# Attention stage of a fused kernel: another order of work on four engines, sinks masked after the turn, one copy moved to VectorE

## Chip, core and metric

One core of a Trainium2 chip. The metric is the time of one execution on the device in microseconds (us), the median of three runs.

## The reference

Three layers follow one another: attention with sinks and a sliding window, a dense layer with a cosine gate, and a top-1 mixture of experts. Only the attention is touched.

```python
# q, k, v: (4, 8, 768, 64); n_sink = 4, window = 128
scores = q @ k.T / sqrt(D)
keep = (key < n_sink) | ((query - key >= 0) & (query - key < window))
a = exp(where(keep, scores, -1e9) - rowmax); a = a / (a.sum() + 1e-9)
attn = a @ v
# then x: (3072, 512) -> dense (512 -> 2048 -> 512) -> 8 experts (512 -> 1024 -> 512)
```

## The kernel before

The 32 heads are taken as 16 pairs. A pair has 6 blocks of 128 queries (QB = 6), one step each; an iteration `it` is two pairs, 12 steps, and there are 8. Since the window is 128, a block of queries sees its own block of keys, the block before, and the sinks: 32 columns of the first keys. The two blocks complement each other: where a key of the own block lies ahead of the query, the same column of the block before is in the window. So both are joined into one block of 128 columns; block 0, which has none before it, takes a filler of -1e30 (`unseen`).

For step n, block n, both heads:

- PE `scores(n)` (L1518, L1519): four products (q by k_hi and k_lo for two heads) into `twin[n % 2]`. It waits for the exponentials of step n-2.
- DVE `join_scores(n)`: one predicated copy into the twin (L1073) and the row maximum (L1075).
- ACT `exponentials(n)`: neg_max (L783) and two exponentials into `probs` (L791).
- PE `turn_probs(n)`, two steps later (TURN_LAG): two transposes (L1527); behind an odd block also `turn_sinks` (L1532), one transpose for the sinks of two blocks, into the third part of `X_BANK`.
- DVE `copy_probs(n)` (L1083): the turned block times the two triangles `halves_of`, which takes the joined block apart again.
- ACT `copy_sinks(m)` for odd m (L798): the turned sinks to `sink_probsT`.
- PE `weigh_window(n)`, three steps later (PV_LAG, L1548): eight products with v (four in block 0), and for odd blocks `weigh_sinks` (L1555), which waits for `copy_sinks`.
- DVE `scale_o(m)` for odd m, four steps later (L1091 to L1096), then PE `turn_o(m)` (L1565) and ACT `stage_x(m)` (L806), five steps later.

Beside this, the next pair's q and k are split into a high and a low part, in four parts: 0 and 2 are halves of q, 1 and 3 halves of k. ACT makes the high part in `split_part` (L777, L779), POOL the low part (L621, L623). POOL also fills the sink columns of k (`fill_sinks`, L606 to L610) ahead of parts 0 and 2, for the k half 1 and 3; ACT's high part of k waits for that fill. The table `PARTS` says in which step of a pair ACT takes which part.

Each engine works through its list in program order. All waits are semaphores written by hand. The waits that matter here:

```python
# PE, turn_sinks(m): x_stage of the group before last
at_least(pe, x_staged, group(it, m) - 1)
# PE, weigh_sinks(m)
pe.wait_ge(sinksT_made, group(it, m) + 1)
# ACT, split_part, for a part of k
act.wait_ge(sinks_filled, 2 * (2 * it + i) + c // 2 + 1)
```

A group is two blocks, so the first one makes turn_sinks(m) wait for stage_x(m-4), which ACT makes in its step m+1, while PE turns the sinks of m in step m+2.

Of the kernel before, what the change touches and what calls it, by code (L numbers as in the profile page):

```python
# [20 lines left out]
U32 = mybir.dt.uint32  # L21
# [18 lines left out]
def build_program(nc, q_twice, k_twice, kT, v, config, w_dense, modality, w_gate, w_gate_rows, modality_bias, w_expert, out):  # L40
# [37 lines left out]
    with ctx:  # L78
# [46 lines left out]
        with ExitStack() as a:  # L125
# [17 lines left out]
            twice_sinks = sb("twice_sinks", [P, 1], where=a)  # L143
            unseen = sb("unseen", [P, WIDE], where=a)
            masks = sb("masks", [P, WIDE + SINK], where=a)
            halves_of = sb("halves_of", [P, 2, P], where=a)

        with ExitStack() as a:
# [227 lines left out]
        def group(it, m):  # L376
            return STEPS // 2 * it + m // 2
# [15 lines left out]

        JOINED = slice(WIDE, 2 * WIDE)

# [7 lines left out]
        KEYS = (0, 0, P + SINK, 2 * P + SINK, 3 * P + 2 * SINK, 4 * P + 2 * SINK)  # L403
        PARTS = ((0,), (), (1,), (2,), (3,), ())
        ORDER = (0, 1, 2, 3, 8, 4, 9, 5, 10, 6, 11, 7, 12, 13, 14, 15)
# [360 lines left out]
        def _(act):  # L766
# [40 lines left out]

            def leave_bank(it, n):
                at = lagged(it, n, TURN_LAG)
                if at and at[1] < STEPS and at[1] % 2 == 1:  # L810
                    copy_sinks(*at)
                at = lagged(it, n, STAGE_LAG)
                if at and at[1] % 2 == 1:
                    stage_x(*at)

            def attention(it, last=False):
                for n in range(STEPS):
                    leave_bank(it, n)
                    exponentials(it, n)
                    if not (last and n >= QB):  # L820
                        for c in PARTS[n % QB]:
                            split_part(*after_pair(it, n // QB), c)
                    elif n - QB < 4:
                        split_dense(n - QB)

            def any_pair(pair):
# [30 lines left out]
            with act.If(narrow == 1):  # L857
# [7 lines left out]
                for n in range(STEPS, STEPS + STAGE_LAG):  # L865
                    if n - STEPS < KD:
                        split_x(0, range(n - STEPS, n - STEPS + 1))
                    leave_bank(ITERS - 1, n)
                act.drain().then_inc(stage1_ends, 1)
# [134 lines left out]
        def _(dve):  # L1004
# [9 lines left out]
            dve.memset(unseen[:, :], UNSEEN).then_inc(masks_made, 1)  # L1014
            dve.memset(twin[1][:, :, 0:SINK], UNSEEN).then_inc(masks_made, 1)
            dve.tensor_scalar(masks[:, 0:SINK], diff[:, 0:SINK], 0.0, None, ALU.is_lt).then_inc(masks_made, 1)
            dve.tensor_scalar(masks[:, SINK:WIDE], diff[:, :], 0.0, None, ALU.is_lt).then_inc(masks_made, 1)
            dve.tensor_scalar(masks[:, WIDE:], diff[:, 0:SINK], 0.0, None, ALU.is_ge).then_inc(masks_made, 1)
            dve.tensor_scalar(halves_of[:, 0, :], diff[:, :], 0.0, None, ALU.is_gt).then_inc(masks_made, 1)
            dve.tensor_scalar(halves_of[:, 1, :], diff[:, :], 0.0, None, ALU.is_le).then_inc(masks_made, 1)  # L1020
            dve.wait_ge(masks_made, 7)
            dve.wait_ge(config_loaded, 16)
# [22 lines left out]
            def make_sink_masks():  # L1045
# [3 lines left out]
                step(dve.tensor_scalar(twice_sinks[HD:, :], twice_sinks[HD:, :], float(HD), None, ALU.add))  # L1049
                dve.tensor_scalar(sink_on[HD:, :], diff_2[HD:, 0:1], twice_sinks[HD:, 0:1], None, ALU.is_lt).then_inc(masks_made, 1)  # L1050

# [8 lines left out]
            def join_scores(it, n):  # L1060

                i, to = n % QB, twin[n % 2]
                if i == 0:
                    into, of, chosen = JOINED, unseen[:, :].unsqueeze(1), masks[:, SINK:]
                elif i == 1:
                    into, of, chosen = JOINED, to[:, :, 0:WIDE], masks[:, 0:WIDE]
                else:
                    own = SINK + WIDE if i % 2 else WIDE
                    into, of, chosen = slice(own, own + P), to[:, :, SINK:WIDE], masks[:, SINK:WIDE]
                shape = [P, 2, WIDE if i < 2 else P]  # L1070
                dve.wait_ge(scores_done, STEPS * it + n + 1)
                dve.sem_inc(carried_dve, 1)
                dve.copy_predicated(to[:, :, into], chosen.bitcast(U32).unsqueeze(1).broadcast_to(shape), of.broadcast_to(shape)).then_inc(scores_joined, 1)  # L1073
                dve.wait_ge(scores_joined, STEPS * it + n + 1)
                dve.tensor_reduce(row_max[:, 2 * n:2 * n + 2], to[:, :, JOINED], AX.X, ALU.max).then_inc(max_made, 1)  # L1075

            def copy_probs(it, m):
# [5 lines left out]
                dve.tensor_tensor(probsT[m % 2][:, first:, :, :], turned.unsqueeze(1).broadcast_to(shape),  # L1083
                                  halves_of[:, first:, :].unsqueeze(2).broadcast_to(shape), ALU.mult).then_inc(probsT_made, 1)

            def scale_o(it, m):
# [16 lines left out]

            def attention_step(it, n):
                at = lagged(it, n, TURN_LAG)
                if at and at[1] < STEPS:
                    copy_probs(*at)
                if n < STEPS:
                    join_scores(it, n)
                at = lagged(it, n, SCALE_LAG)  # L1110
                if at and at[1] % 2 == 1:
                    scale_o(*at)

# [391 lines left out]
        def _(pe):  # L1505

            def scores(it, n):
# [3 lines left out]
                keys = slice(KEYS[i], KEYS[i] + (WIDE if i == 0 else P + WIDE))  # L1511
                cols = JOINED if i == 0 else slice(SINK, 2 * WIDE)
                for h in range(2):
# [109 lines left out]
            with pe.If(narrow == 1):  # L1623
                pe.wait_ge(masks_made, 8)
                pe.wait_ge(sums_made, 8)
# [254 lines left out]
```

## Time and profile before

| | us |
|---|---|
| median of three runs | 1096.53 |
| lowest, highest | 1095.62, 1097.69 |
| time of the profiled execution | 1097.69 |
| its span, first to last instruction | 1095.7 |

The profile is of one execution. Engines are PE (TensorE), PEld (its weight loads), DVE (VectorE), ACT (ScalarE), POOL (GpSimd). A row of a timeline gives the start in us from the span's start, the length, the engine, the line and operation, what it writes and reads with shapes, how many instructions are merged, and in brackets the idle time before it with its releaser. Starts overlap the end of the instruction before them, because engines are pipelined; the distance between two starts is what an instruction costs the queue. The granted TensorE clock was 0.997 of full speed over the span.

### The profile page before, as it was taken

What the parts mean: (1) busy time and instruction counts of PE and PEld (TensorE: products, weight loads), DVE (VectorE), ACT (ScalarE), POOL (GpSimd) and SP (SyncE); (2) the same over time, 40 slices, a digit from 0 to 9 for tenths busy, and PEclk for the clock granted to TensorE, in tenths of its full rate; (3) what the DMA queues carried; (4) which work ended last, traced back from release to release, by engine and by line L of the source; (5) the groups of instructions that cost most, each with busy time, mean ns of one, the idle gap of its engine ahead of it and who ended that gap; (6) DMA issues with size and microseconds to landing.
All of it is one profiled execution on the core that took longest, in us unless ns stands there. A gap on an engine that the chain in (4) does not pass through costs nothing.

```text
span 1095.7 us, 18853 instructions
## 1 busy us (share of the span) xinstructions
PE 1061.4 (97%) x5976; PEld 915.6 (84%) x5977; DVE 692.9 (63%) x1514; ACT 479.4 (44%) x991; POOL 290.4 (27%) x356
## 2 busy tenths in 40 slices
PE   4999999999999999999999999999999999999997
PEld 4999999878888888888888887888789998999986
DVE  5989999766687578658748768867542222522225
ACT  4878888754433343343334344336341122421124
POOL 6878888700000000000000000511333222222223
PEclk9999999999999999999999999999999999999999
DMA  5877777372120020001002001023261101611102
GB/s 164 258 212 210 209 203 225 108 240 74 77 77 1 1 77 1 1 28 50 1 1 77 1 0 40 5 97 117 88 221 51 46 20 40 192 41 55 37 20 96
DMA packets 58507, 94.90 MB, mean 87 GB/s; under 512 B 11598, under 2 KB 40654, under 8 KB 58320
## 3 DMA queue, kind: packets, MB, share of 16 engines
q1 hardware_dynamic: 52240, 79.76, 23.3%
q0 software_dynamic: 6208, 14.40, 4.0%
q8 instruction: 32, 0.52, 0.2%
q14 instruction: 27, 0.22, 0.1%
HBM read 75.06 MB, written 21.69 MB: 88 GB/s over the span
## 4 chain that ended last, share of the span: by engine, by line
PE 89%; DMA 3%; DVE 3%; issue 2%; ACT 1%; POOL 1%; POOLq 0%; DVEq 0%; ACTq 0%; SPq 0%
PE twin L1650 24%; PE twin L1738 13%; PE bank L1666 12%; PE twin L1666 12%; PE twin L1753 11%; PE bank L1548 6%; PE bank L1527 2%; PE twin L1519 2%; PE twin L1518 2%; PE bank L1555 2%; PE bank L1704 1%; DMA xg<-y_scratch,next_ids 1%; PE bank L1565 1%; DMA out<-late,now_ids 1%; DMA raw_k<-k_twice 1%
## 5 line engine op out<-in xcount | busy, mean ns | idle before, releaser
L690 POOL DMA_INDIRECT list_scratch<-entry,slot_i x24 | 26.7, 1112 | 517.2 <-DVE slot_i L1319 506.0
L1650 PE MATMUL twin<-x_hi,w_hi 128*128 128x512 f32 x384 | 152.6, 397 | 1.4 <-DVE g_sb L1229 0.9
L1650 PE MATMUL twin<-x_hi,w_lo 128*128 128x512 f32 x384 | 152.0, 396 | 0.0
L1650 PE MATMUL twin<-x_lo,w_hi 128*128 128x512 f32 x384 | 151.9, 396 | 0.0
L1440 DVE SCALAR_TENSOR_TENSOR g_lo<-twin,g_hi 128x256 fp32r<-128x256 f32 x112 | 47.5, 424 | 163.2 <-ACT g_hi L948 158.1
L1738 PE MATMUL twin<-xg_hi,w_hi 128*128 128x256 f32 x448 | 127.3, 284 | 2.8 <-issue 2.5
L1738 PE MATMUL twin<-xg_hi,w_lo 128*128 128x256 f32 x448 | 126.0, 281 | 1.2 <-issue 1.2
L1738 PE MATMUL twin<-xg_lo,w_hi 128*128 128x256 f32 x448 | 126.8, 283 | 0.0
L948 ACT ACTIVATE g_hi<-twin 128x256 fp32r<-128x256 f32 x112 | 43.0, 384 | 182.2 <-PE twin L1738 177.1
L912 ACT ACTIVATE turns<-turns 128x512 f32<-128x512 f32 x96 | 60.7, 632 | 134.0 <-DVE turns L1222 132.7
L1204 DVE CUSTOM_DVE_ANT_0 whole<-y_sb,raw 128x512 f32<-128x512 f32 x160 | 109.8, 686 | 1.9
L906 ACT ACTIVATE turns<-twin 128x512 f32<-128x512 f32 x96 | 57.2, 596 | 117.8 <-PE twin L1650 117.6
L1220 DVE TENSOR_SCALAR whole<-turns 128x512 f32<-128x512 f32 x96 | 41.3, 430 | 82.6 <-ACT turns L906 79.9
L917 ACT ACTIVATE g_hi<-g_sb 128x512 fp32r<-128x512 f32 x96 | 60.8, 634 | 72.8 <-DVE g_sb L1229 72.1
L1738 PEld LDWEIGHTS twin<-xg_hi,w_hi 128*128 128x128 f32 x448 | 85.0, 190 | 7.7 <-issue 4.0
L1548 PE MATMUL bank<-v_sb,probsT 128*128 128x65 f32 x704 | 90.4, 270 | 0.1
L1650 PEld LDWEIGHTS twin<-x_hi,w_hi 128*128 128x128 f32 x384 | 72.1, 188 | 20.0 <-DVE g_sb L1229 1.3
L1548 PEld LDWEIGHTS bank<-v_sb,probsT 128*128 128x128 f32 x704 | 87.5, 193 | 0.4 <-DMA v_sink<-v_n 0.3
L1738 PEld LDWEIGHTS twin<-xg_lo,w_hi 128*128 128x128 f32 x448 | 85.1, 190 | 3.2
L1650 PEld LDWEIGHTS twin<-x_hi,w_lo 128*128 128x128 f32 x384 | 72.1, 188 | 17.6
L1738 PEld LDWEIGHTS twin<-xg_hi,w_lo 128*128 128x128 f32 x448 | 85.3, 190 | 1.4 <-issue 1.4
L1650 PEld LDWEIGHTS twin<-x_lo,w_hi 128*128 128x128 f32 x384 | 72.2, 188 | 16.9
(213 smaller groups left out, 2542.7 us busy)
## 6 DMA issues: line engine op xcount, KB each, us to landing
raw<-w_expert SPq DMA_DIRECT2D x32, 512.0 KB, 4.9
raw_q<-q_twice SPq DMA_DIRECT2D x32, 384.0 KB, 3.8
raw<-w_dense SPq DMA_DIRECT2D x16, 512.0 KB, 4.6
raw_k<-k_twice SPq DMA_DIRECT2D x16, 448.0 KB, 3.8
raw_k<-k_twice SPq DMA_DIRECT2D x16, 416.0 KB, 4.7
v_sb<-v_n SPq DMA_DIRECT2D x16, 384.0 KB, 4.1
xT_scratch<-x_stage SPq DMA_DIRECT2D x16, 384.0 KB, 3.8
x_raw<-xT_scratch SPq DMA_DIRECT2D x6, 1024.0 KB, 5.1
```

The costliest lines, as they stand in the source:

```text
L906: act.activation(turns[:, :], H_BANK[f % 2][:, :], ACT.Copy, scale=INV_2PI, bias=0.25).then_inc(turns_made, 1)
L912: act.activation(cosine[:, :], frac[:, :], ACT.Sin, scale=TWO_PI).then_inc(cos_made, 1)
L917: act.activation(g_hi[n % 3][:, :], g_sb[:, :], ACT.Copy).then_inc(g_hi_made, 1)
L948: act.activation(h_hi[f % 4], EH_BANK[f % 2][:, 0:TT], ACT.Relu).then_inc(h_hi_made, 1)
L1204: dve.tensor_tensor_reduce(out=dump[:, :], in0=y_sb[:, t, :], in1=gate_rows[:, e, :], scale=1.0, scalar=0.0, op0=ALU.mult, op1=ALU.add, ac ...
L1220: dve.tensor_scalar(whole[:, :], turns[:, :], ROUND, ROUND, ALU.add, ALU.subtract).then_inc(whole_made, 1)
L1440: dve.scalar_tensor_tensor(out=h_lo[f % 4], in0=EH_BANK[f % 2][:, 0:TT], scalar=0.0, in1=h_hi[f % 4].bitcast(F32), op0=ALU.max, op1=ALU.su ...
L1548: last = pe.matmul(O_BANK[m // 2 % 2][:, at:at + HD + 1], probsT[m % 2][:, b, h, :], v_sb[par][:, i - 1 + b, (HD + 1) * h:(HD + 1) * (h + 1)],
L1650: last = pe.matmul(H_BANK[f % 2][:, :], a[:, w], b[:, k, :], start=x == 0, stop=x == 3 * KD - 1)
L1666: last = pe.matmul(Y_BANK[t][:, :], a[n % 3][:, t * P:(t + 1) * P], b[:, w], start=f == 0 and x == 0, stop=f == FB1 - 1 and x == 2)
L1738: last = pe.matmul(EH_BANK[f % 2][:, 0:TT], a[:, w], b[:, k, :], start=x == 0, stop=x == 3 * KD - 1)
L1753: last = pe.matmul(EY_BANK[j][:, :], a[f % 4][:, j * P:(j + 1) * P], b[:, w], start=f == 0 and x == 0, stop=f == FB2 - 1 and x == 2)
```

## The change

- **PE**: scores(n) is issued ahead of turning block n-2; weigh_sinks ahead of turn_o; turn_o no longer waits for the sink copy.
- **ACT**: `leave_bank` (sink copy and x_stage) becomes `attention_end` and stands behind the step's exponentials and split_part, where it stood ahead of them. The sink copy of the first group of a pair (blocks 0 and 1) is left to DVE. `PARTS` changes.
- **DVE**: scale_o, join_scores, copy_probs is the new order within a step, and behind it the sink copy of the first group, as a product with a mask `sink_part`.
- **The masks**: the sink columns of blocks 0 and 1 are no longer masked in the scores (joins of 160 columns a head) but by `sink_part` after the turn; all joins have 128 columns a head. The scores' place in the twin moves by 32 columns.

```diff
-        JOINED = slice(WIDE, 2 * WIDE)
+        JOINED = slice(P, P + WIDE)
-        PARTS = ((0,), (), (1,), (2,), (3,), ())
+        PARTS = ((0,), (1,), (), (2,), (), (3,))
 # ACT
-            def leave_bank(it, n):
+            def attention_end(it, n):
                 at = lagged(it, n, TURN_LAG)
-                if at and at[1] < STEPS and at[1] % 2 == 1:
+                if at and at[1] < STEPS and at[1] % 2 == 1 and at[1] % QB > 1:
                     copy_sinks(*at)
...
                 for n in range(STEPS):
-                    leave_bank(it, n)
                     exponentials(it, n)
                     if not (last and n >= QB):
                         for c in PARTS[n % QB]:
                             split_part(*after_pair(it, n // QB), c)
                     elif n - QB < 4:
                         split_dense(n - QB)
+                    attention_end(it, n)
 # DVE, setup
-            dve.memset(twin[1][:, :, 0:SINK], UNSEEN).then_inc(masks_made, 1)
-            dve.tensor_scalar(masks[:, 0:SINK], diff[:, 0:SINK], 0.0, None, ALU.is_lt).then_inc(masks_made, 1)
-            dve.tensor_scalar(masks[:, SINK:WIDE], diff[:, :], 0.0, None, ALU.is_lt).then_inc(masks_made, 1)
-            dve.tensor_scalar(masks[:, WIDE:], diff[:, 0:SINK], 0.0, None, ALU.is_ge).then_inc(masks_made, 1)
+            dve.tensor_scalar(prior[:, :], diff[:, :], 0.0, None, ALU.is_lt).then_inc(masks_made, 1)
...
+            dve.tensor_scalar(sink_part[0:HD, :], diff_2[0:HD, :], 2.0, None, ALU.is_ge).then_inc(masks_made, 1)
+            dve.tensor_scalar(sink_part[HD:, :], diff_2[HD:, :], float(HD + 1), None, ALU.is_le).then_inc(masks_made, 1)
...
+                dve.tensor_scalar(sink_part[:, :], sink_part[:, :], sink_on[:, 0:1], None, ALU.mult).then_inc(masks_made, 1)
+                dve.wait_ge(masks_made, 7)
 # DVE, join_scores
-                if i == 0:
-                    into, of, chosen = JOINED, unseen[:, :].unsqueeze(1), masks[:, SINK:]
-                elif i == 1:
-                    into, of, chosen = JOINED, to[:, :, 0:WIDE], masks[:, 0:WIDE]
-                else:
-                    own = SINK + WIDE if i % 2 else WIDE
-                    into, of, chosen = slice(own, own + P), to[:, :, SINK:WIDE], masks[:, SINK:WIDE]
-                shape = [P, 2, WIDE if i < 2 else P]
+                own = slice(WIDE, WIDE + P) if i % 2 else slice(P, 2 * P)
+                from_block = to[:, :, 0:P] if i else unseen[:, :].unsqueeze(1).broadcast_to(both)
 # DVE, new
+            def copy_sinks(it, m):
+                g = group(it, m)
+                dve.wait_ge(sinks_turned, g + 1)
+                at_least(dve, sinks_weighed, g)
+                dve.tensor_tensor(sink_probsT[:, :], X_BANK[:, 2 * P:3 * P], sink_part[:, :], ALU.mult).then_inc(sinksT_made, 1)
...
             def attention_step(it, n):
+                at = lagged(it, n, SCALE_LAG)
+                if at and at[1] % 2 == 1:
+                    scale_o(*at)
+                if n < STEPS:
+                    join_scores(it, n)
                 at = lagged(it, n, TURN_LAG)
                 if at and at[1] < STEPS:
                     copy_probs(*at)
-                if n < STEPS:
-                    join_scores(it, n)
-                at = lagged(it, n, SCALE_LAG)
-                if at and at[1] % 2 == 1:
-                    scale_o(*at)
+                    if at[1] % QB == 1:
+                        copy_sinks(*at)
 # PE
-            def turn_o(it, m, last=False):
+            def turn_o(it, m):
                 g = group(it, m)
                 pe.wait_ge(o_scaled, g + 1)
-                if not last:
-                    pe.wait_ge(sinksT_made, g + 2)
...
             def attention_step(it, n):
                 turn = lagged(it, n, TURN_LAG)
-                turn = turn if turn and turn[1] < STEPS else None
-                if turn:
+                if turn and turn[1] < STEPS:
                     turn_probs(*turn)
-                if n < STEPS:
-                    scores(it, n)
-                if turn and turn[1] % 2 == 1:
-                    turn_sinks(*turn)
+                    if turn[1] % 2 == 1:
+                        turn_sinks(*turn)
                 at = lagged(it, n, PV_LAG)
-                at = at if at and at[1] < STEPS else None
-                if at:
+                if at and at[1] < STEPS:
                     weigh_window(*at)
-                staged = lagged(it, n, STAGE_LAG)
-                if staged and staged[1] % 2 == 1:
-                    turn_o(*staged, last=n == STEPS + STAGE_LAG - 1)
-                if at and at[1] % 2 == 1:
-                    weigh_sinks(*at)
+                    if at[1] % 2 == 1:
+                        weigh_sinks(*at)
+                at = lagged(it, n, STAGE_LAG)
+                if at and at[1] % 2 == 1:
+                    turn_o(*at)
 
             def attention(it):
                 for n in range(STEPS):
+                    scores(it, n)
                     attention_step(it, n)
```

## Rows read from the trace of the kernel before

**Rows 1.** The page's first line, and one stretch of the table by stretches.

```profile
span 1095.7 us, 18853 instructions
...
116.00:128.00 12.00, 12.00 (x97) 11.55 (x97) 11.16 (x28) 9.94 (x29) 9.97 (x11) 1.00 0.70 208
```

**Rows 2.** Chain that ended last, 100 to 160 us: start, length, what; three pairs apart.

```profile
118.75 0.39 PE bank L1548 x4
...
154.51 0.39 PE bank L1548 x4
```

**Rows 3.** Timeline of PE, 128 to 131 us.

```profile
128.18 1.00 PE L1548 MATMUL bank<-v_sb,probsT 128*128 128x65 f32 x8
129.01 0.39 PE L1565 MATMUL bank<-ident,o_sb 128*128 128x128 f32 x2
129.24 0.60 PE L1555 MATMUL bank<-v_sink,sink_probsT 128*128 128x260 f32 x2
129.68 0.39 PE L1527 MATMUL bank<-ident,probs 128*128 128x128 f32 x2
...
130.45 0.27 PE L1532 MATMUL bank<-ident,probs 128*128 128x128 f32 x1
130.56 0.56 PE L1548 MATMUL bank<-v_sb,probsT 128*128 128x65 f32 x4
130.95 0.47 PE L1527 MATMUL bank<-ident,probs 128*128 128x128 f32 x2
```

**Rows 4.** Timeline of ACT, 118 to 124 us.

```profile
118.72 0.95 ACT L777 ACTIVATE k_hi<-raw_k 128x896 fp32r<-128x896 f32 x1
119.56 0.37 ACT L798 ACTIVATE sink_probsT<-bank,sink_on 128x128 f32<-128x128 f32 x1
119.81 0.21 ACT L783 ACTIVATE neg_max<-row_max 128x2 f32<-128x2 f32 x1
120.13 0.70 ACT L791 ACTIVATE probs<-twin,neg_max 128x160 f32<-128x160 f32 x2
120.71 0.84 ACT L779 ACTIVATE qs<-raw_q 128x768 fp32r<-128x768 f32 x1
121.44 0.38 ACT L806 ACTIVATE x_stage<-bank 128x256 f32<-128x256 f32 x1
...
123.24 0.90 ACT L777 ACTIVATE k_hi<-raw_k 128x832 fp32r<-128x832 f32 x1 [0.25 <-POOL raw_k L610]
```

**Rows 5.** Timeline of POOL, 119 to 130 us.

```profile
119.87 2.10 POOL L621 TENSOR_TENSOR k_lo<-raw_k,k_hi 128x896 fp32r<-128x896 f32 x1 [0.60 <-ACT k_hi L777]
...
123.49 1.82 POOL L623 TENSOR_TENSOR qs<-raw_q,qs 64x768 fp32r<-64x768 f32 x1 [0.28 <-POOL raw_k L610]
125.48 2.01 POOL L621 TENSOR_TENSOR k_lo<-raw_k,k_hi 128x832 fp32r<-128x832 f32 x1 [0.17 <-POOL qs L623]
...
128.65 0.45 POOL L610 TENSOR_TENSOR raw_k<-raw_k,first_sink 128x124 f32<-128x124 f32 x1 [0.18 <-POOL raw_k L607]
```

**Rows 6.** Timeline of DVE, 121 to 125 us.

```profile
121.00 0.42 DVE L1073 COPY_PREDICATED twin<-masks,twin 128x256 f32<-128x256 uint32 x1
121.45 0.49 DVE L1075 TENSOR_REDUCE row_max<-twin 128x2 f32<-128x320 f32 x1
121.86 0.68 DVE L1083 TENSOR_TENSOR probsT<-bank,halves_of 128x512 f32<-128x512 f32 x1
122.49 0.43 DVE L1073 COPY_PREDICATED twin<-masks,twin 128x256 f32<-128x256 uint32 x1
...
124.70 0.97 DVE L1073 COPY_PREDICATED twin<-masks,unseen 128x320 f32<-128x320 uint32 x1
```

**Rows 7.** Timeline of PE's weight loads at the stage's end.

```profile
201.96 0.14 PEld L1532 LDWEIGHTS bank<-ident,probs 128*128 128x128 f32 x1 [0.23 <-ACT x_stage L806]
```

**Rows 8.** A group by form (busy, mean ns), and the first filler join in the timeline.

```profile
L1083 DVE TENSOR_TENSOR probsT<-bank,halves_of 128x256 f32<-128x256 f32 x16 | 6.6, 414 | 0.8 <-PE bank L1527 0.8
...
14.41 1.89 DVE L1073 COPY_PREDICATED twin<-masks,unseen 128x320 f32<-128x320 uint32 x1 [1.36 <-PE twin L1519]
```

More of the change, by code:

```diff
@@ L143, in build_program @@
             twice_sinks = sb("twice_sinks", [P, 1], where=a)
-            unseen = sb("unseen", [P, WIDE], where=a)
-            masks = sb("masks", [P, WIDE + SINK], where=a)
+            unseen = sb("unseen", [P, P], where=a)
+            prior = sb("prior", [P, P], where=a)
             halves_of = sb("halves_of", [P, 2, P], where=a)
+            sink_part = sb("sink_part", [P, P], where=a)
         with ExitStack() as a:
@@ L867, in _ @@
                         split_x(0, range(n - STEPS, n - STEPS + 1))
-                    leave_bank(ITERS - 1, n)
+                    attention_end(ITERS - 1, n)
                 act.drain().then_inc(stage1_ends, 1)
@@ L1014, in _ @@
             dve.memset(unseen[:, :], UNSEEN).then_inc(masks_made, 1)
-            dve.memset(twin[1][:, :, 0:SINK], UNSEEN).then_inc(masks_made, 1)
-            dve.tensor_scalar(masks[:, 0:SINK], diff[:, 0:SINK], 0.0, None, ALU.is_lt).then_inc(masks_made, 1)
-            dve.tensor_scalar(masks[:, SINK:WIDE], diff[:, :], 0.0, None, ALU.is_lt).then_inc(masks_made, 1)
-            dve.tensor_scalar(masks[:, WIDE:], diff[:, 0:SINK], 0.0, None, ALU.is_ge).then_inc(masks_made, 1)
+            dve.tensor_scalar(prior[:, :], diff[:, :], 0.0, None, ALU.is_lt).then_inc(masks_made, 1)
             dve.tensor_scalar(halves_of[:, 0, :], diff[:, :], 0.0, None, ALU.is_gt).then_inc(masks_made, 1)
             dve.tensor_scalar(halves_of[:, 1, :], diff[:, :], 0.0, None, ALU.is_le).then_inc(masks_made, 1)
-            dve.wait_ge(masks_made, 7)
+            dve.tensor_scalar(sink_part[0:HD, :], diff_2[0:HD, :], 2.0, None, ALU.is_ge).then_inc(masks_made, 1)
+            dve.tensor_scalar(sink_part[HD:, :], diff_2[HD:, :], float(HD + 1), None, ALU.is_le).then_inc(masks_made, 1)
+            dve.wait_ge(masks_made, 6)
             dve.wait_ge(config_loaded, 16)
@@ L1049, in make_sink_masks @@
                 step(dve.tensor_scalar(twice_sinks[HD:, :], twice_sinks[HD:, :], float(HD), None, ALU.add))
-                dve.tensor_scalar(sink_on[HD:, :], diff_2[HD:, 0:1], twice_sinks[HD:, 0:1], None, ALU.is_lt).then_inc(masks_made, 1)
+                step(dve.tensor_scalar(sink_on[HD:, :], diff_2[HD:, 0:1], twice_sinks[HD:, 0:1], None, ALU.is_lt))
+                dve.tensor_scalar(sink_part[:, :], sink_part[:, :], sink_on[:, 0:1], None, ALU.mult).then_inc(masks_made, 1)
+                dve.wait_ge(masks_made, 7)
             def make_sum_columns():
@@ L1060, in join_scores @@
             def join_scores(it, n):
-                i, to = n % QB, twin[n % 2]
-                if i == 0:
-                    into, of, chosen = JOINED, unseen[:, :].unsqueeze(1), masks[:, SINK:]
-                elif i == 1:
-                    into, of, chosen = JOINED, to[:, :, 0:WIDE], masks[:, 0:WIDE]
-                else:
-                    own = SINK + WIDE if i % 2 else WIDE
-                    into, of, chosen = slice(own, own + P), to[:, :, SINK:WIDE], masks[:, SINK:WIDE]
-                shape = [P, 2, WIDE if i < 2 else P]
+                i, both = n % QB, [P, 2, P]
+                to = twin[n % 2]
                 dve.wait_ge(scores_done, STEPS * it + n + 1)
                 dve.sem_inc(carried_dve, 1)
-                dve.copy_predicated(to[:, :, into], chosen.bitcast(U32).unsqueeze(1).broadcast_to(shape), of.broadcast_to(shape)).then_inc(scores_joined, 1)
+                own = slice(WIDE, WIDE + P) if i % 2 else slice(P, 2 * P)
+                from_block = to[:, :, 0:P] if i else unseen[:, :].unsqueeze(1).broadcast_to(both)
+                dve.copy_predicated(to[:, :, own], prior[:, :].bitcast(U32).unsqueeze(1).broadcast_to(both), from_block).then_inc(scores_joined, 1)
                 dve.wait_ge(scores_joined, STEPS * it + n + 1)
@@ L1511, in scores @@
                 keys = slice(KEYS[i], KEYS[i] + (WIDE if i == 0 else P + WIDE))
-                cols = JOINED if i == 0 else slice(SINK, 2 * WIDE)
+                cols = slice(P, P + WIDE) if i == 0 else slice(0, P + WIDE)
                 for h in range(2):
@@ L1623, in _ @@
             with pe.If(narrow == 1):
-                pe.wait_ge(masks_made, 8)
+                pe.wait_ge(masks_made, 7)
                 pe.wait_ge(sums_made, 8)
```

## Prediction

> **What bounds the kernel now.** I began with the span [rows 1] and the table by stretches of 12 us, of which one stands in [rows 1]. The diff touches the attention stage alone (about 13 to 213 us of the span); what follows it is dense work of TensorE, which starts when this stage ends, so what the stage gains or loses moves the end one for one. In the stretch shown PE never looks idle, and DVE, ACT and POOL are each busy 9.9 to 11.2 of 12 us: four engines nearly full, so busy time alone decides nothing. Next the chain that ended last: it runs through PE in this stage, and its one group of four window products per pair of heads (block 0 has no previous block) marks the pairs [rows 2]. From 118.75 to 154.51 are three pairs: 11.92 us a pair, 16 pairs.
>
> Last the timelines of the four engines, read by starts, since a start-to-start distance is what an instruction costs its queue. PE [rows 3]: eight window products 0.83, two turns of o 0.23, weighing the sinks 0.44, turning two probability blocks and four score products 0.77 (0.22 and 0.55), turning the sinks 0.11, four window products 0.39. A pair is 6 x 0.77 + 3 x 0.11 + 5 x 0.83 + 0.39 + 3 x (0.23 + 0.44) = 11.50 us. So PE waits only about 0.4 of 11.92 us: it bounds the stage, and the others follow closely. The end of a PE instruction lies about 0.17 after the start of the next one (1.00 long, 0.83 to the next, [rows 3]).
>
> ACT [rows 4]: maximum to exponentials 0.32; the two exponentials to the next instruction 0.58; k_hi 0.84 to the next (the narrower half is 0.90 long instead of 0.95, so 0.79); sink copy 0.37 long, 0.25 to the next; qs 0.73; x_stage 0.38 long. DVE [rows 6]: join to reduce 0.45, reduce 0.49 long and 0.41 to the next, copy_probs 0.63. POOL [rows 5]: its k_lo starts 0.20 after ACT's k_hi ends (118.72 + 0.95 against 119.87); from the start of k_lo for part 3 to the end of the next pair's sink fill 125.48 to 129.10 = 3.62. For another hop from engine to engine I take 0.04, next to the 0.03 from the end of a join to its reduce [rows 6].
>
> **The change, part by part.** Below, step n is the position in a pair, (n) a block, and the clock is zero when PE has issued scores(5).
>
> *PE's order.* scores(n) now stands ahead of turning block n-2, and weighing the sinks ahead of turn_o. No PE work is added. The wait of turn_o on the sink copy costs nothing to drop: weigh_sinks, now in front of it, waits for the same copy.
>
> *ACT's order.* This is the costly part. The sink copy of block n-3 (made in ACT's step n-1) now stands behind that step's exponentials and behind split_part, and PARTS puts parts 1, 2, 3 exactly in the odd steps 1, 3, 5, where the copies are. Scores(5) end at 0.17, DVE joins at 0.21, reduces 0.66 to 1.15, neg_max 1.19, exponentials 1.51, k_hi of part 3 2.09, sink copy(3) 2.88 to 3.25, PE 3.29. PE wants that copy after turn(3), turn_sinks(3), weigh_window(2), scores(0), turn(4), weigh_window(3): 0.22 + 0.11 + 0.83 + 0.55 + 0.22 + 0.83 = 2.76. So it is 0.5 late. In step 3 the copy is DVE's (below).
>
> *PARTS, and POOL.* Part 3's k_hi ends at 2.99; POOL's k_lo starts at 3.19 and its sink fill for the next pair ends at 3.19 + 3.62 = 6.81. ACT's k_hi of part 1, in step 1, needs that fill: 6.85. Before, it stood in step 2 and had a step more. Then sink copy(5) 7.69 to 8.06, PE weighs the sinks at 8.10. A PE that has waited restarts with its weight load (0.14 for one turn of the sinks, [rows 7]); I add 0.10. Then weigh 0.44, turn_o 0.23, scores(3) 0.55: 9.42. From there PE is fed: turn 0.22, turn_sinks 0.11, four window products 0.39, scores(4) 0.55, turn 0.22, weigh_window 0.83, weigh_sinks 0.44, turn_o 0.23, scores(5) 0.55 = 3.54, so 12.96. That is the new period of a pair.
>
> *x_stage behind the exponentials.* turn_sinks(m) waits for x_stage(m-4), which ACT now makes behind the exponentials of the step before; that wait is already seen at the stage's end, 0.23 long [rows 7]. In step 4: join(3) at 9.42 + 0.21 = 9.63, reduce 10.08, copy_probs 10.49, DVE's new sink copy 11.12, join(4) 11.35, reduce 11.80, neg_max 12.33, exponentials 12.65, x_stage 13.23 to 13.61, PE 13.65, which is 0.69 on the new clock where PE was there at 0.22. From it scores(0) end at 0.69 + 0.10 + 0.11 + 0.83 + 0.55 + 0.17 = 2.45, join(0) 2.49, reduce 2.82, neg_max 3.35, exponentials 3.67, qs of part 0 4.25, x_stage 4.98 to 5.36, PE turns sinks(5) at 5.40, and is ready to weigh them at 5.40 + 0.10 + 0.11 + 0.83 + 0.55 + 0.22 + 0.83 = 8.04. That is within 0.1 of the 8.10 above: two chains of one length, and 12.96 doesn't hang on one of them alone.
>
> *DVE.* The sink copy of blocks 0 and 1 is new there. Its shape stands in no row; the nearest is the 128x256 product, 0.41 long [rows 8], so it costs between nothing and 0.41; I take 0.23, a little over half. At 0.41 the second chain grows by 0.18 and the pair by about 0.1. The joins of blocks 0 and 1 go from 320 to 256 columns. Block 0's reads mask and filler both from SBUF, and here a stall hides: it took 0.97 and ended 0.36 after POOL's qs (124.70 + 0.97 = 125.67; 123.49 + 1.82 = 125.31) [rows 5, 6]; the first one took 1.89 [rows 8]. I read it as 0.36 of work, 0.30 for 256 columns, and a wait for POOL. In the new order POOL has finished qs of part 2 well before 2.49 (its k_hi partner is split two steps later than it) and starts k_lo at 3.19, so 0.30 + 0.03 stands in the chain above. Kept at 0.97 it would bring PE to 8.68 instead of 8.10: 0.58 a pair, 9 us.
>
> The Trainium skill, SBUF — State Buffer, section "Who interferes with whom", says that a DVE instruction with two SBUF inputs and a GpSimd instruction that reads SBUF exclude each other for the whole instruction, and the one issued later blocks. By that rule the join costs its bare work here, the 0.30 already in the sum; by the trace's mean length instead the sum would be the 9 us higher. The trace agrees with it (0.36 after POOL's end).
>
> *Setup.* Smaller masks go, sink_part comes, and one more step stands ahead of the first scores. It lies under the first join, which waits for POOL anyway (1.89, [rows 8]); uncovered it would be some 0.4. I add nothing.
>
> **The sum.** 12.96 - 11.92 = 1.04 a pair, times 16 = 16.6 us. The last pair (it splits dense weights instead) and the first are taken like the others. The profiled execution's own time is 1097.69, 1.16 above the median of the three; 1097.69 + 16.6 = 1114.3 on its count, 1096.53 + 16.6 = 1113.1 on the median's.
>
> **Rivals.**
> - *The copies come in time after all* (faster). DVE now joins directly behind scores, with no copy_probs ahead, and a join loses its wait for POOL. If ACT runs so far ahead that sink copy and x_stage are there when wanted, PE runs at its 11.50: -0.42 x 16 = -6.7, 1089.8. It decides if ACT gains 0.5 us in every odd step. For it: the wait for POOL goes. Against: ACT can't start exponentials before the scores of the same step end, and 3.29 against 2.76 counts no queue at all ahead of it.
> - *Only the sink copies bite.* The x_stage chain is shorter than read and k_hi of part 1 finds its fill: 2 x (3.29 + 0.10 - 2.76) = 1.26 on 11.50 is 12.76, +0.84 x 16 = 13.4, 1110. If PE's own slack takes half, 1103.
> - *Join(0) meets k_lo* (much slower). If join(0) slips from 2.49 past 3.19, POOL has the lock until 3.19 + 2.01 = 5.20, and the join ends at 5.50 instead of 2.79: 2.7 later. PE then weighs at 10.7, +2.6 a pair more, 42 us: 1155. It decides at a slip of 0.7. For it: the filler join's lengths of 0.97 and 1.89. Against: the phase worked out above. The rule of the Trainium skill's SBUF — State Buffer page cited above is of the same kind: in the other order of issue the join is the one that blocks.
> - *Little changes*: the lost and won waits cancel, 1096.5.
>
> **How the numbers follow.** Forecast 0.66 (own range 1106 to 1121), only the sink copies 0.14, join(0) meets k_lo 0.06, copies in time 0.10, little change 0.04. The time is the forecast's, 1113.1. Low end 1101: half of the second rival's. High end 1123: the forecast with join(0) at its old length (+9). Outside lie 0.10 + 0.04 + 0.06. Slower by over 0.2% (2.2 us, about what a measurement can tell from no change here) 0.86, the same 0.04, faster 0.10.
>
> **What would show it.** In the profile after: a pair some 13.0 us long by the four-product marks; PE waiting for sink_probsT ahead of the sink products about twice a pair, 0.1 to 0.6 each; PE waiting for x_stage ahead of turning the sinks, about 0.5, in steps 5 and 1; ACT's k_hi of part 1 waiting for POOL's fill; the 128x256 join with the filler near 0.30; POOL idle over 1 us a pair ahead of k_lo of part 3. Wrong would be a PE without waits and a pair of 11.5, or filler joins of over 1 us.

## The result, and the profile after

The changed kernel takes 1126.05 us (median of four runs, 1124.81 to 1127.89), the kernel before on the same chip 1096.59: a ratio of 1.027, interval 1.0249 to 1.029. That is 29.5 us slower. The prediction said slower, by 16.6; the time lies 3 us above the upper end of its range.

The page's first line, and the same stretch of the table by stretches as in [rows 1] (start and end, length, then busy time of PE, PEld, DVE, ACT, POOL with counts, clock, DMA share, GB/s):

```profile
span 1126.0 us, 18846 instructions
...
116.00:128.00 12.00, 11.13 (x86) 10.31 (x86) 10.02 (x24) 8.13 (x24) 8.13 (x10) 1.00 0.58 158
```

Every engine is less busy than in [rows 1]: ACT 8.13 instead of 9.94, POOL 8.13 instead of 9.97, and PE now shows 0.9 us of idle time. No engine is busy all the time any more. The marks of [rows 2] in the timeline of PE:

```profile
106.41 0.59 PE L1553 MATMUL bank<-v_sb,probsT 128*128 128x65 f32 x4
...
148.06 0.56 PE L1553 MATMUL bank<-v_sb,probsT 128*128 128x65 f32 x4
```

Three pairs in 41.65 us, 13.88 a pair instead of 11.92. 1.96 x 16 = 31.4, which is the loss and a little more. Forecast was 12.96. One pair in the timeline of PE, the starts to set beside [rows 3] and the prediction's clock (its zero, scores(5) issued, is 124.39 here):

```profile
124.39 0.39 PE L1532 MATMUL bank<-ident,probs 128*128 128x128 f32 x2
...
126.40 0.48 PE L1532 MATMUL bank<-ident,probs 128*128 128x128 f32 x2 [0.21 <-ACT probs L792]
...
127.79 0.71 PE L1560 MATMUL bank<-v_sink,sink_probsT 128*128 128x260 f32 x2
...
129.08 0.39 PE L1532 MATMUL bank<-ident,probs 128*128 128x128 f32 x2
129.66 0.33 PE L1537 MATMUL bank<-ident,probs 128*128 128x128 f32 x1 [0.19 <-ACT x_stage L807]
...
132.54 0.71 PE L1560 MATMUL bank<-v_sink,sink_probsT 128*128 128x260 f32 x2
...
133.84 0.39 PE L1532 MATMUL bank<-ident,probs 128*128 128x128 f32 x2
...
135.06 0.29 PE L1524 MATMUL twin<-k_lo,qs 128*128 128x288 f32 x1
135.85 0.48 PE L1532 MATMUL bank<-ident,probs 128*128 128x128 f32 x2 [0.50 <-DVE probsT L1080]
...
138.26 0.39 PE L1532 MATMUL bank<-ident,probs 128*128 128x128 f32 x2
```

PE weighs the sinks of block 3 at 127.79, 3.40 on the clock (forecast 3.29), turns the sinks of block 5 at 5.27 (5.40), weighs them at 8.15 (8.10), and has issued scores(3) at 133.84, 9.45 (9.42). So far the times hold. From scores(3) to scores(5) the forecast was 3.54, and the trace has 138.26 - 133.84 = 4.42. The hole is at 135.85: PE turns block 2 only when DVE has made copy_probs(1). DVE, in the same stretch:

```profile
134.15 0.43 DVE L1070 COPY_PREDICATED twin<-prior,twin 128x256 f32<-128x256 uint32 x1
134.61 0.49 DVE L1072 TENSOR_REDUCE row_max<-twin 128x2 f32<-128x320 f32 x1
135.02 0.68 DVE L1080 TENSOR_TENSOR probsT<-bank,halves_of 128x512 f32<-128x512 f32 x1
135.62 0.28 DVE L1087 TENSOR_TENSOR sink_probsT<-bank,sink_part 128x128 f32<-128x128 f32 x1
```

join(3), its reduce, then copy_probs(1), over at 135.70; PE turns at 135.85. Both use the one bank that turned blocks go through, and PE waits for it by a semaphore that stands in both kernels and is not among the waits listed ahead of the prediction:

```python
# PE, turn_probs(m): the copy of block m-1 has left the bank
at_least(pe, probsT_made, STEPS * it + m)
```

In the order before, copy_probs was the first of a DVE step. Of the two late things on ACT, the timeline of ACT (with [rows 4]):

```profile
126.59 0.89 ACT L778 ACTIVATE k_hi<-raw_k 128x832 fp32r<-128x832 f32 x1
127.37 0.37 ACT L799 ACTIVATE sink_probsT<-bank,sink_on 128x128 f32<-128x128 f32 x1
...
131.28 0.95 ACT L778 ACTIVATE k_hi<-raw_k 128x896 fp32r<-128x896 f32 x1
132.14 0.35 ACT L799 ACTIVATE sink_probsT<-bank,sink_on 128x128 f32<-128x128 f32 x1
```

And POOL, for its wait ahead of k_lo of part 3 (with [rows 5]):

```profile
127.68 1.96 POOL L622 TENSOR_TENSOR k_lo<-raw_k,k_hi 128x832 fp32r<-128x832 f32 x1 [2.62 <-ACT k_hi L778]
...
130.80 0.45 POOL L611 TENSOR_TENSOR raw_k<-raw_k,first_sink 128x124 f32<-128x124 f32 x1 [0.18 <-POOL raw_k L608]
```

The fill ends at 131.25 and ACT's k_hi of part 1 starts at 131.28, when it was forecast (6.89 on the clock for 6.85). But the trace doesn't show ACT waiting for it there: the exponentials ahead of it started at 130.71, and the 0.57 from there to k_hi is what they cost anyway. The fill and ACT's own queue come to the same time.

### The profile page after: what moved, and what is told of

It reads as the page before. It is cut to its first block, busy times and chain, and to the rows that moved or that the text cites. A ratio compares the mean times of both kernels' runs of the same rounds, so it can differ in the third digit from the quotient of the medians.

```text
span 1126.0 us, 18846 instructions
## 1 busy us (share of the span) xinstructions
PE 1077.3 (96%) x5976; PEld 921.6 (82%) x5977; DVE 696.8 (62%) x1530; ACT 477.5 (42%) x975; POOL 286.0 (25%) x356
## 4 chain that ended last, share of the span: by engine, by line
PE 83%; DVE 6%; issue 4%; ACT 4%; DMA 1%; POOL 1%; DVEq 0%; ACTq 0%; POOLq 0%; SPq 0%
PE twin L1650 24%; PE twin L1738 14%; PE twin L1753 12%; PE bank L1666 12%; PE twin L1666 12%; PE bank L1553 2%; PE bank L1560 2%; DVE twin L1070 2%; DVE row_max L1072 1%; PE twin L1523 1%; PE twin L1524 1%; ACT probs L792 1%; PE bank L1704 1%; PE bank L1532 1%; DMA raw_k<-k_twice 1%
## 5 line engine op out<-in xcount | busy, mean ns | idle before, releaser
L691 POOL DMA_INDIRECT list_scratch<-entry,slot_i x24 | 26.7, 1112 | 517.4 <-DVE slot_i L1324 506.1
L1239 DVE TENSOR_TENSOR g_lo<-g_sb,g_hi 128x512 fp32r<-128x512 f32 x96 | 66.4, 692 | 30.7 <-ACT g_hi L918 25.1
```

What stands on the lines that cost most here:

```text
L1239: dve.tensor_tensor(g_lo[n % 3][:, :], g_sb[:, :], g_hi[n % 3][:, :].bitcast(F32), ALU.subtract).then_inc(g_lo_made, 1)
```

## The experiments

Thirteen kernels, all timed beside the kernel before on the same chip. The change falls into five parts that can be set one by one: the masks with the DVE sink copy, PE's order, DVE's order, ACT's order, PARTS. Pair lengths are from the four-product marks, 3 to 10 pairs each.

| kernel | time | before | ratio (interval) | pair |
|---|---|---|---|---|
| the change | 1126.05 | 1096.59 | 1.027 (1.0249 to 1.029) | 13.88 |
| e1, copy_probs(1) ahead of join(3) | 1124.09 | 1095.89 | 1.0256 (1.0237 to 1.0276) | 13.68 |
| e2, scale_o last | 1129.45 | 1095.89 | 1.0307 (1.0282 to 1.0332) | 14.06 |
| e3, ACT's order undone | 1115.3 | 1095.89 | 1.0177 (1.0156 to 1.0199) | 13.26 |
| e4, PARTS undone | 1147.27 | 1095.89 | 1.0467 (1.0448 to 1.0485) | 15.37 |
| e5, sink copy early | 1118.65 | 1095.86 | 1.0203 (1.0182 to 1.0224) | 13.36 |
| e6, x_stage early | 1129.27 | 1095.86 | 1.031 (1.0292 to 1.0328) | 14.18 |
| e7, ACT's order and PARTS undone | 1121.23 | 1095.86 | 1.0226 (1.0209 to 1.0243) | 13.60 |
| e8, masks alone | 1096.82 | 1095.9 | 1.0009 (0.9996 to 1.0023) | 11.90 |
| e9, ACT's order and PARTS alone | 1138.49 | 1095.9 | 1.0396 (1.0378 to 1.0414) | 14.77 |
| e10, PE's and DVE's orders alone | 1121.79 | 1095.9 | 1.0241 (1.0223 to 1.0258) | 13.75 |
| e11, masks and PE's order | 1100.08 | 1095.9 | 1.0043 (1.0028 to 1.0059) | 12.28 |
| e12, DVE's order undone | 1200.38 | 1095.69 | 1.0936 (1.0892 to 1.098) | 19.14 |
| e13, e1 and x_stage early in step 4 | 1117.49 | 1097.03 | 1.0199 (1.0174 to 1.0225) | 13.43 |

**e1.** Theory A was read off the profile after: the turn of block 2 waits for copy_probs(1). Theory B was that scale_o ahead of the joins delays everything.

```diff
 # DVE, attention_step
+                early = n % QB == 3
+                at = lagged(it, n, TURN_LAG)
+                if early and at and at[1] < STEPS:
+                    copy_probs(*at)
                 if n < STEPS:
                     join_scores(it, n)
-                at = lagged(it, n, TURN_LAG)
                 if at and at[1] < STEPS:
-                    copy_probs(*at)
+                    if not early:
+                        copy_probs(*at)
```

> The changed kernel, with DVE making copy_probs(1) ahead of join(3) in step 3 of a pair (nothing else). Theory A, the wait that the prediction left out: PE's turn of block 2 waits for copy_probs(1), because both use the same bank, and in step 4 only four window products lie between; about 0.7 us a pair. Then a pair goes from 13.87 to about 13.15 and the kernel from 1126 to about 1114.5. Theory B, the surplus comes from scale_o standing ahead of the joins: nothing gained, 1126 or a little more, since join(3) is made later.

1124.09: 2 us better at most, and the interval of its ratio overlaps the change's; the pair is 0.20 shorter. By its number that is theory B's outcome, and theory A's 1114.5 is missed by far. The trace says why. From scores(3) to scores(5) it takes 3.89 instead of 4.42 (131.89 to 135.78, and 3.79 in every second pair), as theory A has it. But the rest of the pair grew from 9.45 to 9.86 (122.03 to 131.89):

```profile
122.03 0.47 PE L1536 MATMUL bank<-ident,probs 128*128 128x128 f32 x2
123.16 0.33 PE L1541 MATMUL bank<-ident,probs 128*128 128x128 f32 x1 [0.67 <-ACT x_stage L807]
...
127.98 0.33 PE L1541 MATMUL bank<-ident,probs 128*128 128x128 f32 x1 [0.57 <-ACT x_stage L807]
...
131.89 0.39 PE L1536 MATMUL bank<-ident,probs 128*128 128x128 f32 x2
...
135.78 0.39 PE L1536 MATMUL bank<-ident,probs 128*128 128x128 f32 x2
```

Turning the sinks now waits for x_stage twice, up to 0.67: join(3) comes later, with it the exponentials of steps 3 and 4, and x_stage stands behind them. The wait was taken away and a new one took its place.

**e2.**

```diff
 # DVE, attention_step
-                at = lagged(it, n, SCALE_LAG)
-                if at and at[1] % 2 == 1:
-                    scale_o(*at)
                 if n < STEPS:
                     join_scores(it, n)
...
                         copy_sinks(*at)
+                at = lagged(it, n, SCALE_LAG)
+                if at and at[1] % 2 == 1:
+                    scale_o(*at)
```

> The changed kernel with scale_o behind join and copy_probs on DVE. Theory A: joins of odd steps start 0.1 us earlier and copy_probs(1) too, about 0.3 a pair, 1121. Theory B (scale_o ahead of the joins is what made the pair 0.9 longer than forecast): 1112.

1129.45, some 3 us worse (0.18 a pair): theory B falls. The gain of theory A did not come either. The stretch from scores(3) to scores(5) is 4.42 as in the change; the rest of the pair is 9.48 and 9.76 by turns, and in the longer ones PE waits 0.78 for x_stage ahead of turning the sinks of block 5. Why x_stage comes so late there stays open.

**e3.** `attention_end(it, n)` moved back ahead of `exponentials(it, n)`.

```diff
                 for n in range(STEPS):
+                    attention_end(it, n)
                     exponentials(it, n)
...
                         split_dense(n - QB)
-                    attention_end(it, n)
```

> The changed kernel with sink copy and x_stage ahead of the exponentials again on ACT. Theory A: PE's waits for sink copy and x_stage go, but turning blocks 4, 0 and 2 still waits for DVE's copy_probs, some 0.4, 0.4 and 0.75 a pair on 11.5: about 13.0 a pair, 1112. Rival C (ACT's order is the whole loss): PE is fed, 11.5 to 11.9 a pair, 1090 to 1097.

1115.3, 13.26 a pair: 3 us above theory A's number, and rival C falls. What is left is the turns' wait: from scores(3) to scores(5) it is 4.43 here too. The profile names ACT there, but the exponentials that this turn needs, those of block 2, were over at 127.94; what ended right before the turn is the copy out of its bank.

```profile
128.23 0.29 PE L1524 MATMUL twin<-k_lo,qs 128*128 128x288 f32 x1
129.00 0.48 PE L1532 MATMUL bank<-ident,probs 128*128 128x128 f32 x2 [0.48 <-ACT probs L792]
...
133.44 0.47 PE L1532 MATMUL bank<-ident,probs 128*128 128x128 f32 x2 [0.21 <-ACT probs L792]
```

DVE's copy_probs there ran 128.18 to 128.86.

**e4.**

```diff
-        PARTS = ((0,), (1,), (), (2,), (), (3,))
+        PARTS = ((0,), (), (1,), (2,), (3,), ())
```

> The changed kernel with the old table PARTS. Theory A: the sink copies come in time, but now every even step has a split ahead of x_stage, which comes 3.3 us after the scores where PE wants it after 2.55: about 14.0 a pair, 1128, so no gain. Rival D (the loss is the sink copies behind the splits and the fill behind k_lo, the first of the two chains of the prediction): about 13.0 a pair, 1112.

1147.27, 19 us above theory A's number: rival D falls, since with the sink copies free of splits the kernel is 21 us worse. Theory A had the place right and the size far too small. x_stage is late in all three even steps:

```profile
122.75 0.33 PE L1537 MATMUL bank<-ident,probs 128*128 128x128 f32 x1 [0.87 <-ACT x_stage L807]
...
127.82 0.33 PE L1537 MATMUL bank<-ident,probs 128*128 128x128 f32 x1 [0.77 <-ACT x_stage L807]
...
132.37 0.33 PE L1537 MATMUL bank<-ident,probs 128*128 128x128 f32 x1 [0.69 <-ACT x_stage L807]
```

With x_stage behind the exponentials, the new table is what makes the change bearable: it takes the splits out of steps 2 and 4.

**e5 and e6.** Only the sink copy, or only x_stage, ahead of the exponentials:

```diff
 # e5; in e6 the two calls change places
                 for n in range(STEPS):
+                    sinks_end(it, n)
                     exponentials(it, n)
...
-                    attention_end(it, n)
+                    stage_end(it, n)
```

> The changed kernel with only the sink copy ahead of the exponentials again; x_stage stays behind. Two chains of nearly one length: alone this gives little, about 13.55 a pair, 1121. If the sink copies are the only chain: 1112.

> The changed kernel with only x_stage ahead of the exponentials again; the sink copy stays behind. By the two chains about 13.7 a pair, 1123.5. If x_stage is the only chain: 1112.

1118.65 and 1129.27. The sink copies are worth 7 us alone, a little more than expected; x_stage alone is worth nothing and costs 3 to 4. Both together give 10 (e3). In e6 PE still waits for the copy, and the turns' wait is still there:

```profile
126.34 0.47 PE L1539 MATMUL bank<-ident,probs 128*128 128x128 f32 x2 [0.21 <-ACT probs L792]
...
132.78 0.70 PE L1567 MATMUL bank<-v_sink,sink_probsT 128*128 128x260 f32 x2 [0.43 <-ACT sink_probsT L799]
```

**e7.** e3 and e4 together.

> The changed kernel with ACT's order and the table PARTS both as before; what is left of the change is PE's order, DVE's order and the masks. Theory A: PE's turns wait for copy_probs, about 13.0 a pair, 1112. Rival C (ACT is the whole loss): 1090 to 1097.

1121.23. ACT wholly as before, and 25 us are still lost: rival C is dead. PE waits in every even step, and of its waits between 60 and 200 us the profile lists no other:

```profile
122.70 0.47 PE L1532 MATMUL bank<-ident,probs 128*128 128x128 f32 x2 [0.21 <-DVE probsT L1080]
...
127.50 0.48 PE L1532 MATMUL bank<-ident,probs 128*128 128x128 f32 x2 [0.28 <-DVE probsT L1080]
...
131.91 0.48 PE L1532 MATMUL bank<-ident,probs 128*128 128x128 f32 x2 [0.49 <-DVE probsT L1080]
```

It is 6 us behind e3, which differs by PARTS alone. The filler join is 0.46 long on average in e3 and 1.24 here (groups by form, busy and mean ns); it now overlaps POOL's qs of part 2 (it ran 122.64 to 123.95, and qs ended at 123.65). Whether this is what makes the 6 us was not tested:

```profile
L1070 DVE COPY_PREDICATED twin<-prior,unseen 128x256 f32<-128x256 uint32 x16 | 19.9, 1243 | 2.6 <-PE twin L1524 1.4
```

**e8.** From here the parts are added to the kernel before. The masks alone; `copy_sinks` on DVE stands behind join(3).

```diff
-        JOINED = slice(WIDE, 2 * WIDE)
+        JOINED = slice(P, P + WIDE)
...
-                if at and at[1] < STEPS and at[1] % 2 == 1:
+                if at and at[1] < STEPS and at[1] % 2 == 1 and at[1] % QB > 1:
...
                 if n < STEPS:
                     join_scores(it, n)
+                if at and at[1] < STEPS and at[1] % QB == 1:
+                    copy_sinks(*at)
```

> The kernel before with the mask part alone: joins of 128 columns, sink_part, the sink copy of blocks 0 and 1 on DVE behind join(3); all orders and PARTS as before. The filler join loses part of its wait for POOL (0.97 down to 0.3 to 0.7), DVE gains the copy (0.2 to the next). Theory A, the masks cost nothing and the orders are the whole loss: 1091 to 1096. Rival E, the copy on DVE costs on the path: above 1098.

1096.82 against 1095.9, ratio 1.0009 with an interval that holds 1: no difference. Rival E falls, and the masks are no gain either, though the filler join went down from 0.90 to 0.65 on average.

**e9.** ACT's order and PARTS alone, on the kernel before (`attention_end` is `leave_bank` under its new name).

```diff
-        PARTS = ((0,), (), (1,), (2,), (3,), ())
+        PARTS = ((0,), (1,), (), (2,), (), (3,))
...
                 for n in range(STEPS):
-                    leave_bank(it, n)
                     exponentials(it, n)
...
                         split_dense(n - QB)
+                    attention_end(it, n)
```

> The kernel before with ACT's new order and the new PARTS alone. Sink copies and x_stage come late as in the prediction, about 1.0 a pair by its two chains, but no turn waits for copy_probs, since DVE makes it ahead of the join: 1112 to 1115. If the surplus beyond the forecast belongs to ACT's order and not to DVE's: 1122 or more.

1138.49: a clear miss of 1112 to 1115, and worse than the whole change. By its number this is the outcome for a surplus that belongs to ACT's order. But the surplus of this kernel is made of other waits than the changed kernel's, and PE doesn't wait for copy_probs here. Two things were left out of that expectation. The third sink copy is on ACT here and also stands behind a split, and in PE's old order turn_o waits for the copy too:

```profile
119.67 0.33 PE L1532 MATMUL bank<-ident,probs 128*128 128x128 f32 x1 [0.59 <-ACT x_stage L806]
...
127.25 0.44 PE L1565 MATMUL bank<-ident,o_sb 128*128 128x128 f32 x2 [0.77 <-ACT sink_probsT L798]
...
132.19 0.43 PE L1565 MATMUL bank<-ident,o_sb 128*128 128x128 f32 x2 [0.71 <-ACT sink_probsT L798]
```

ACT's order with PARTS is the costliest part by itself, 43 us. On top of the other three it adds only 4 to 5 (e7 against the change). That PE's and DVE's orders bring the joins earlier and ask for the copies later would explain this; it was not tested by itself.

**e10 and e11.** PE's and DVE's orders alone; and the masks with PE's order, DVE's order left as before. Their edits are the parts of the diff under "PE" and under "DVE", shown ahead of the prediction; e11 takes the masks and the DVE sink copy as in e8.

> The kernel before with PE's and DVE's new orders alone, the old masks, ACT's order and PARTS as before. Theory A: the turns wait for copy_probs in three steps of a pair, as in the run with ACT and PARTS undone (13.6 a pair there); with the old filler join no better: 1119 to 1125. Rival: these orders are harmless and it was the masks: 1096.

> The kernel before with the masks and PE's new order; DVE makes copy_probs ahead of the join as before. If the turns' wait comes from DVE's order (copy_probs behind the join), it is gone: the pair falls from 13.6 to about 11.9, 1094 to 1100. If PE's order is what costs: about 1115 to 1120.

1121.79 is as expected, and the rival that these orders are harmless (1096) falls. 1100.08 is at the edge of what was expected, with 12.28 a pair for 11.9. e7 and e11 differ by DVE's order alone: 1121.23 against 1100.08, so 21 us for join and scale_o ahead of copy_probs. PE's order with the masks costs 4.

**e12.** The changed kernel with DVE's order as before. This asks whether the 21 us can be had back inside the change.

> The changed kernel with DVE's order as before (copy_probs ahead of the join, scale_o last); PE's and ACT's orders, PARTS and masks as changed. Theory A says the parts work on one another: the turn of block 2 no longer waits, but each join now stands behind copy_probs, which waits for a turn that PE issues behind the scores, so it starts 0.4 to 0.8 later and ACT's late sink copies and x_stage come that much later: 14.5 to 15.2 a pair, 1137 to 1149. Rival F, DVE's order is a loss of its own (it cost 21 us with ACT's order as before): 1105 to 1112.

1200.38: far from both numbers, and above theory A's. The wait that theory A named is there: copy_probs waits for a turn that PE issues behind the scores, here for 3.01. The timeline of DVE:

```profile
134.47 0.69 DVE L1080 TENSOR_TENSOR probsT<-bank,halves_of 128x512 f32<-128x512 f32 x1 [3.01 <-PE bank L1532]
```

But neither number reckoned with TensorE's clock. The line of the core, with the mean granted clock:

```profile
core 0: 1203.4 us, clock 0.943
```

And the timeline of PE:

```profile
129.83 1.81 PE L1553 MATMUL bank<-v_sb,probsT 128*128 128x65 f32 x8
131.44 1.18 PE L1560 MATMUL bank<-v_sink,sink_probsT 128*128 128x260 f32 x2
...
135.69 1.00 PE L1553 MATMUL bank<-v_sb,probsT 128*128 128x65 f32 x8
136.53 0.66 PE L1560 MATMUL bank<-v_sink,sink_probsT 128*128 128x260 f32 x2
...
139.75 0.33 PE L1537 MATMUL bank<-ident,probs 128*128 128x128 f32 x1 [1.53 <-ACT x_stage L807]
```

Eight window products took 1.61 from start to start at 129.83 and 0.84 at 135.69: the clock went between its two levels, 1.2 and 2.4 GHz. Over 14 to 100, 100 to 200 and 200 to 309 us the granted clock was 0.86, 0.79 and 0.77 of full speed, and 0.99 behind that. An estimate from these figures: at most 0.14 x 86 + 0.21 x 100 + 0.23 x 109 = 58 us of the profiled execution's 1205.3 are the clock, so at full clock it would have taken 1147 or more. That keeps rival F (1105 to 1112) fallen; how far theory A's 1137 to 1149 would have held isn't shown.

**e13.** e1 had traded one wait for another. Here both are taken away.

```diff
 # besides the edit of e1, on ACT
                 for n in range(STEPS):
+                    if n % QB == 4:
+                        stage_end(it, n)
                     exponentials(it, n)
...
+                if n % QB != 4 or n >= STEPS:
+                    stage_end(it, n)
```

> The changed kernel with copy_probs(1) ahead of join(3) in step 3 on DVE, and in step 4 x_stage ahead of the exponentials on ACT; all else as changed. If the surplus over the forecast is the turn's wait, kept alive by the x_stage chain: 3.54 to 3.7 us from scores(3) to scores(5) and 9.45 for the rest, 13.0 to 13.2 a pair, 1112 to 1116, the prediction's own number. If a third chain holds the stage: over 13.5 a pair, 1121 or more.

1117.49, 13.43 a pair: between the two numbers, nearer to the first. From scores(3) to scores(5) it is 3.78 (128.41 to 132.19), and the rest 9.65 (118.76 to 128.41), where it was 9.45:

```profile
118.76 0.48 PE L1545 MATMUL bank<-ident,probs 128*128 128x128 f32 x2
...
122.34 0.71 PE L1573 MATMUL bank<-v_sink,sink_probsT 128*128 128x260 f32 x2
...
128.41 0.39 PE L1545 MATMUL bank<-ident,probs 128*128 128x128 f32 x2
...
132.19 0.48 PE L1545 MATMUL bank<-ident,probs 128*128 128x128 f32 x2
```

So 0.64 of the 0.88 that was missing is this wait, shown by taking it away: 9 us less than the change, each against its own kernel before. What x_stage early in step 4 gives without e1's edit was not run. 0.2 came back elsewhere, since DVE's maximum of step 5 came later, and with it the sink weighing (3.58 on the clock instead of 3.40).

## Why the prediction was wrong

- **What bounds the kernel, PE's 11.50 a pair.** Nothing spoke against it; no run averages less than 11.90 a pair. Its split of 0.77 into 0.22 for a turn and 0.55 for the scores is misread: in [rows 3] the turn costs 0.14 (129.68 to 129.82) and the scores 0.63 (129.82 to 130.45). The sum is the same in the old order, but not in the new one, see below.
- **Sink copies late behind split_part.** Right in place and time: 3.40 for 3.29 and 8.15 for 8.10. The 0.11 is scale_o, which stands ahead of join(5) on DVE and was not counted: the join started at 0.32 on the clock instead of 0.21. Undoing the late copies alone gives 7 us (e5).
- **k_hi of part 1 waits for POOL's fill.** Right in time, but not shown as the cause: 0.03 after the fill, and no later than the exponentials ahead of it allow (130.71 plus their usual 0.57). The profile's longest chain reaches this k_hi through join(1) and its exponentials and not through POOL. So two chains of one length meet there, and the prediction had worked out one of them. Only in e5, where ACT is early, does the fill end last, and ACT waits 0.16 for it.
- **x_stage behind the exponentials.** Right at block 5: 5.27 for 5.40. At block 3 PE turned the sinks at 124.61, 0.22, with no wait where 0.69 was forecast, because the missing wait below had already made PE late. e1 took that one away and x_stage's wait of 0.67 appeared.
- **The step that failed: "From there PE is fed: turn 0.22, turn_sinks 0.11, four window products 0.39, scores(4) 0.55, turn 0.22 ... = 3.54".** It isn't fed. The second turn shares its bank with copy_probs(1), which the change put behind join and reduce on DVE, and this wait was put at nothing. The prediction dated that copy itself: it starts at 10.49, and with the 0.68 of [rows 6] it ends at 11.17 on its clock; PE's turn of block 2 falls at 9.42 + 0.22 + 0.11 + 0.39 + 0.55 = 10.69. The numbers stood in the text and were never held against each other; with its 0.04 for the hop and 0.10 for the restart they give a wait of 0.62 a pair, 10 us, and 1123.

  Measured were 4.42 for 3.54: 0.88 x 16 = 14.1, and 16.6 + 14.1 = 30.7 against 29.5 measured. In every kernel that keeps copy_probs(1) behind join(3) this stretch is 4.41 to 4.44, whatever ACT, PARTS and the masks do (the change, e2, e3, e5, e6, e7, e10; only e4 has 4.63, with a wait for x_stage in it). With the copy ahead of the join it is 3.78 in e11 and e13 and 3.8 to 3.9 in e1. So the wait is worth 0.64 of the 0.88.

  PE's instructions by themselves are another 0.14: the sum of 3.54 is 3.68 with the costs that the trace shows in the new order (scores 0.62, weighing the sinks 0.50, turn of o 0.14, four window products 0.41, eight 0.84). In the steps with eight window products the same wait is 0.2 to 0.3 (e7), in the change hidden behind that for the sink copies. What the wait costs the kernel is less than its length: without it x_stage's chain is next, 0.2 a pair behind (e1).
- **DVE's sink copy.** 0.28 long, 0.20 to the next, for 0.23. No cost in time with the masks alone (e8).
- **The filler join, 0.30.** It ran alone, as forecast, and was 0.43 long (126.35 to 126.78 in the timeline of DVE). The 0.36 between POOL's end and the join's end [rows 5, 6] isn't the whole work. It was not on the longest chain. The 0.97 taken for its old length is one join; all sixteen average 0.90 in the kernel before.
- **PE's order costs nothing.** It costs 3 to 4 us (e11 against e8). Behind a turn of o the four score products cost 0.62 and the turn behind them 0.22 (133.22 to 133.84 to 134.06), 0.84 for the 0.77 of the old order, while a turn of o went down from 0.23 to 0.14.
- **Rivals.** "Copies in time" and "little changes" fell by the result itself, "only the sink copies bite" by e5, where the sink copies are early and 23 us are still lost; e7 shows that 25 us are lost with ACT wholly as before. Join(0) did not meet k_lo in the changed kernel (0.43 long), but in e7 it was 1.24 on average.

The direction was forecast and the two ACT chains were dated to about 0.1 us; the loss was put at 16.6 instead of 29.5 us because of the one wait left out and, for a smaller part, PE's costs in the new order. What stays open: why x_stage comes later with scale_o last (e2), and how the loss divides between waits that are each a few tenths apart.

## What to carry to other kernels

When four in-order queues are all nearly full, list every wait of every instruction that is moved, the waits for a free buffer too, and date both sides of each; a wait left out is a chain left out. Prices of parts don't add up: ACT's order with PARTS cost 43 us alone and 4 to 5 on top of the others. Taking away the wait that the profile shows can return little, because the next chain is a few tenths behind; undo two at once before calling a theory dead.

## What the runs showed of the hardware

- The predicated copy with both inputs in SBUF waits for POOL's instruction: 0.43 long where POOL was idle, 1.24 on average in e7, 1.62 in e12 with the row below, in an otherwise equal instruction. In e12 it ended 0.29 after POOL's k_lo (143.84), in e7 0.30 after POOL's qs (123.65). The Trainium skill, SBUF — State Buffer, "Who interferes with whom", says that a DVE instruction with two SBUF inputs contends with a GpSimd instruction that reads SBUF, and that the order of issue decides which of the two blocks. These rows agree: POOL's k_lo had started at 141.89, ahead of the join.

```profile
142.51 1.62 DVE L1070 COPY_PREDICATED twin<-prior,unseen 128x256 f32<-128x256 uint32 x1
```

- TensorE's granted clock did not stay at full speed in e12, whose PE waits for x_stage 28 times in the attention stage, 42 us in all and up to 2.8 us at a time: 0.943 to 0.954 over the span in its four executions, against 0.992 to 0.999 in those of all other kernels. Before one such fall PE had waited 1.54 us for x_stage, until 119.50; the eight products from 119.67 still took 0.81, those from 121.49 took 1.60.
- After a wait a pair of transposes costs 0.32 to the next start instead of 0.22 (135.85 to 136.17 in the changed kernel, against 133.84 to 134.06), which is the 0.10 that the prediction had estimated.
